# A table of differences on one core: VectorE's subtraction against two products of TensorE into one sum

## What is computed

```python
for t in range(S):
    m_new = np.maximum(f_gate[:, :, t] + m, i_gate[:, :, t])
    f_stab = np.exp(f_gate[:, :, t] + m - m_new)
    i_stab = np.exp(i_gate[:, :, t] - m_new)
    C = f_stab[..., None, None] * C + i_stab[..., None, None] * np.einsum('bhd,bhe->bhde', vt, kt)
    n = f_stab[..., None] * n + i_stab[..., None] * kt
    h_tilde = np.einsum('bhde,bhe->bhd', C, qt)
    denom = np.maximum(np.abs(np.einsum('bhd,bhd->bh', n, qt)[:, :, None]), 1.0)
    y[:, :, t] = o * h_tilde / denom            # o: sigmoid of o_gate
# then, on 1536 tokens of 320 values:
x = rms_norm(y) ; x = (silu(x @ w_gate) * (x @ w_val)) @ w_out      # 320 -> 1536 -> 320
x = leaky_relu(x @ w_in) @ w_out                                    # 320 -> 2048 -> 320
```

## Time and profile before

| | us |
|---|---|
| median of 3 executions | 440.17 (439.88 to 440.44) |
| the profiled execution | 440.19 |
| its span on the core | 438.5 |
| TensorE busy | 429.8 (98%) |
| VectorE busy | 226.3 (52%) |
| ScalarE busy | 193.3 (44%) |
| GpSimd busy | 91.0 (21%) |

### The profile page before, as it was taken

How to read it: one execution, slowest core, us unless ns; L and a number is a source line. 1 busy time by engine, 2 the same in 40 slices (tenths; PEclk the granted TensorE clock), 3 DMA queues, 4 the chain that set the end, 5 groups by cost and what they waited for, 6 DMA issues and landing times.

```text
span 438.5 us, 8229 instructions
## 1 busy us (share of the span) xinstructions
PE 429.8 (98%) x3237; PEld 377.7 (86%) x3237; DVE 226.3 (52%) x439; ACT 193.3 (44%) x428; POOL 91.0 (21%) x97
## 2 busy tenths in 40 slices
PE   7999999999999999999999999999999999999997
PEld 5889999999788888878888888989999999999996
DVE  8856656775466555456433335353333333533534
ACT  4867753665262535235333226553343343333332
POOL 1798852212111111002333004430000000000000
PEclk9999999999999999999999999999999999999999
DMA  7887623431202410001222102300000000100101
GB/s 213 279 294 257 215 86 124 126 121 51 78 27 98 131 47 0 1 1 33 66 67 66 34 1 67 100 0 1 0 1 0 1 1 1 44 17 0 61 0 60
DMA packets 10692, 30.42 MB, mean 69 GB/s; under 512 B 1296, under 2 KB 3264, under 8 KB 10656
## 3 DMA queue, kind: packets, MB, share of 16 engines
q1 hardware_dynamic: 10656, 29.92, 21.4%
HBM read 27.90 MB, written 2.01 MB: 68 GB/s over the span
## 4 chain that ended last, share of the span: by engine, by line
PE 82%; issue 6%; POOL 4%; DMA 4%; DVE 3%; ACT 1%; SPq 0%; POOLq 0%; DVEq 0%
PE gate_ps L1166 22%; PE value_ps L1166 22%; PE out_ps L1243 9%; PE out_ps L1205 9%; PE turn_ps L1243 6%; PE out_ps L1209 3%; PE c_ps L1243 3%; PE turn_ps L1131 3%; POOL w_sb L483 2%; DMA raw<-in_w 2%; PE turn_ps L1092 1%; DMA att_sb<-in_tok 1%; PE turn_ps L1109 1%; PE c_ps L1121 1%; DMA y_acc<-in_first_gates 1%
## 5 line engine op out<-in xcount | busy, mean ns | idle before, releaser
L1166 PE MATMUL value_ps<-x_hi,w_sb 128*128 128x512 f32 (+1 forms) x280 | 68.6, 367 | 0.5 <-DVE h_lo L929 0.5
L1166 PE MATMUL gate_ps<-x_hi,w_sb 128*128 128x512 f32 (+1 forms) x280 | 68.8, 368 | 0.2
L1166 PEld LDWEIGHTS gate_ps<-x_hi,w_sb 128*128 128x128 f32 x280 | 47.4, 191 | 8.2 <-DVE x_odd L895 1.1
L1166 PEld LDWEIGHTS value_ps<-x_hi,w_sb 128*128 128x128 f32 x280 | 47.7, 191 | 7.4 <-DVE h_lo L929 0.7
L908 DVE SCALAR_TENSOR_TENSOR act_buf<-act_buf,gate_ps 128x512 f32<-128x512 f32 (+1 forms) x46 | 26.2, 569 | 48.1 <-ACT act_buf L619 47.9
L934 DVE TENSOR_TENSOR h_lo<-hid,h_hi 128x512 fp32r<-128x512 f32 x48 | 33.2, 692 | 33.7 <-ACT h_hi L638 33.7
L633 ACT ACTIVATE h_hi<-value_ps 128x512 fp32r<-128x512 f32 (+1 forms) x46 | 23.0, 500 | 58.4 <-DVE value_ps L915 58.2
L1205 PE MATMUL out_ps<-h_hi,w_sb 128*128 128x512 f32 (+1 forms) x184 | 48.2, 348 | 0.0
L638 ACT ACTIVATE h_hi<-hid 128x512 fp32r<-128x512 f32 x48 | 30.3, 632 | 37.6 <-DVE hid L922 36.5
L619 ACT ACTIVATE act_buf<-gate_ps 128x512 f32<-128x512 f32 (+1 forms) x46 | 23.1, 501 | 49.3 <-PE gate_ps L1166 49.1
L1243 PE MATMUL out_ps<-w_sb,h_hi 128*128 128x320 f32 x192 | 43.0, 309 | 0.2 <-DVE h_lo L934 0.2
(11 more groups left out here) (148 smaller groups left out, 797.5 us busy)
## 6 DMA issues: line engine op xcount, KB each, us to landing
raw<-in_w SPq DMA_DIRECT2D x12, 544.0 KB, 4.6
att_sb<-in_tok SPq DMA_DIRECT2D x12, 484.0 KB, 4.8
raw<-in_w SPq DMA_DIRECT2D x16, 352.0 KB, 3.0
expo<-decay_scratch SPq DMA_DIRECT2D x10, 512.0 KB, 5.3
att_sb<-in_qk SPq DMA_DIRECT2D x24, 160.0 KB
out_y<-y_acc SPq DMA_DIRECT2D x12, 160.0 KB, 1.9
consts_sb<-in_consts SPq DMA_DIRECT2D x1, 129.5 KB, 2.7
y_acc<-in_first_gates SPq DMA_DIRECT2D x1, 112.0 KB, 2.6
```

Of the source, the lines that this page charges most:

```text
L1166: last = nc.tensor.matmul(ps[:, 0:n], lhs, rhs, start=(j == 0), stop=(j == len(xs) - 1))
```

## The change

It makes a matrix `minus_unit`, the 16x16 unit matrix times -1, on ScalarE. Line 968 goes. On TensorE `difference` takes the place of the second `table`: for each of the five blocks a product with the unit matrix starts a sum and a product of `stab` with `minus_unit` ends it, so the difference is made while the blocks are turned. The wait for `a_done` 4 goes, and one for `minus_set` comes. Block 2 of the weights is loaded before the decays are written out, and `hi_weights(2)` stands before `square(0)`.

```diff
+            minus_unit = sb(first, "minus_unit", [P, NG])
...
@@ SP
             load_raw(1, W1RAW, w1[1, :, :])
+            load_raw(2, W1RAW, w1[2, :, :])
             sp.wait_ge(a_done, 3)
             sp.dma_start(sums[:, 1:, :], by_time[:, 1:, :]).then_inc(scratch_out, 16)
-            load_raw(2, W1RAW, w1[2, :, :])
             sp.wait_ge(scratch_out, 16)
             load_decays(2)
@@ ACT
+            act.wait_ge(consts_in, 16)
+            nc.scalar.activation(minus_unit[0:NG, :], ident_sb[0:NG, 0:NG], ACT.Copy, scale=-1.0).then_inc(minus_set, 1)
             act.wait_ge(tab_ps, 1)
...
             hi_weights(1)
+            hi_weights(2)
             square(0)
-            hi_weights(2)
             square(1)
@@ DVE
-            nc.vector.tensor_tensor(ig[0:NG, rest], ig[0:NG, rest], m, ALU.subtract).then_inc(a_done, 1)
@@ PE
+            def difference(ps, a, b, t0, t1):
+                pe.wait_ge(minus_set, 1)
+                for t in range(t0, t1):
+                    cols = ps[:, (t - t0) * NG:(t - t0 + 1) * NG]
+                    tok = slice(t * P, (t + 1) * P)
+                    nc.tensor.matmul(cols, a[0:NG, tok], ident_sb[0:NG, 0:NG], start=True, stop=False)
+                    last = nc.tensor.matmul(cols, b[0:NG, tok], minus_unit[0:NG, :], start=False, stop=True)
+                last.then_inc(tab_ps, 1)
...
             table(later_a_ps, acum, 1, SEQ_TILES)
-            pe.wait_ge(a_done, 4)
-            table(later_c_ps, ig, 1, SEQ_TILES)
+            difference(later_c_ps, ig, stab, 1, SEQ_TILES)
             update_state(0)
```

More of the change, by code:

```diff
@@ L143, in build @@
             unseen = sb(first, "unseen", [P, P], BF16)
-            used = 4 * (2 * ATT + EXPO * H * P + 2 * H * DV + 6 * DM + 16 + 2 * H + 2 * PAIRS * DV + 3 * TILES * H
+            minus_unit = sb(first, "minus_unit", [P, NG])
+            used = 4 * (2 * ATT + EXPO * H * P + 2 * H * DV + 6 * DM + 16 + NG + 2 * H + 2 * PAIRS * DV + 3 * TILES * H
                         + TILES * PAIRS + 3 * H + 8) + 4 * P
@@ L227, in build @@
         masks_set = sem("masks_set")
+        minus_set = sem("minus_set")
         rows_set = sem("rows_set")
```

## The result

In the comparison, 22 executions of each kernel on the same chips, the kernel before took 440.34 us (median; 439.69 to 440.88) and the changed one **441.59 us** (440.21 to 444.33). The ratio is 1.0042, with a 95% interval of 1.0028 to 1.0056: slower, by 1.25 us, near the 1.4 us forecast. It is a near hit by luck, for a wrong reason, and the 22 times already say so: none lies between 441.89 and 443.42. They fall apart by their mean granted clock. For the kernel before, the clocks on record are those of the 116 executions that were measured beside the experiments; its 22 executions above have none.

A forecast was written before the change was run, and what follows sets the result against it. It took the prologue before `gate(0)` as bound by TensorE and the VectorE/ScalarE path almost together, with a gapless TensorE run behind. Products +1.76 less 0.23 and 0.13 idle gave +1.4; 440.19 + 1.4 = 441.6 us, range 440.1 to 442.4.

The forecast's parts named there:

- Products for transposes: TensorE's second table: five transposes go, ten products (20 records at 0.117 us) come, +1.76 us.
- rival C: The new products are dear: near +4.0 us on TensorE, less 0.36 idle, giving 443.8 us; chance 0.03.
- What is covered: TensorE before `turn(1)`: idle 0.23 us and about 0.13 of turns' waits absorb part of 1.76, leaving +1.4 us.
- rival A: The clock rises sooner relative to `gate(0)`, giving back some or all of the loss (440.9; 439.5 at best); chance 0.19.
- The clock: TensorE's rise from 1.2 to 2.4 GHz, 3.4 us after `gate(0)` starts, shifts along with it and costs nothing.
- Line 968 and the load: Dropping VectorE's subtraction: nothing, at most 0.35 us gained; block 2's load ahead of the decays: nothing.
- Transfers: Decays written near 16.2 us, tile 2's rows landing near 19.7, masked at 20.90: cover 1.2 us, cost nothing.
- The rounding of block 2: On ScalarE ahead of `square(0)`: `normalise(0)` slips 0.1 us at most, covered by 1.4 us; costs 0.1 without cover.
- Rival D: Later tile 2 rows or later blocks reach ScalarE late and hold `h_hi`: up to 1 us more, 442.6; chance 0.06.

The follow-up runs named there:

- the products alone: The changed kernel with block 2's load and rounding back in their old places: 440.81 us, ratio 1.0033.
- filler: The changed kernel with four wide bf16 products, later overwritten, added in TensorE's idle stretches before the table: 443.57 us, ratio 1.0068.

## Why the prediction came out right, and where it was wrong

**Products for transposes: the mis-sized term.** I chose 0.117 us a record "since weight width and moving width both match", from a row of transposes. Measured are 0.213 at 1.2 GHz and 0.112 at 2.4, against 0.117 and 0.06 for a transpose: about 1.8 times at either level. What such a product costs was in a row that I had, line 1092 at 0.23, and I set it aside because it moves 128 columns where these move 16. That width did not matter. A still nearer row stands in the profile of before, a float32 product with a weight of 16x128, at 1.2 GHz:

```profile
6.19 0.42 PE L1074 MATMUL c_ps<-y_acc,consts_sb 16*128 16x128 f32 x1
...
6.83 0.42 PE L1074 MATMUL c_ps<-y_acc,consts_sb 16*128 16x128 f32 x1
```

Three steps of one record lie between them: (6.83 - 6.19) / 3 = 0.213 us, the new records' price. To be a float32 product is not enough: `update_state`'s records are float32 products as well and need 0.049, with weights of 40 columns in place of 128. At 1.2 GHz the term is 20 x 0.213 - 0.59 = +3.7, in place of +1.76. This was rival C, which I gave 0.03 with the words "no row with 16 moving columns is that slow": no row there was a product. Its 443.8 us is what 9 of the 22 executions show (443.88).

The rule that I had set aside fares better. The Trainium skill (FP8 and Floating Point Precision, section TensorE Precision Notes) counts four passes for true FP32. I worked out an estimate of 4.68 us for the ten products from it and set it aside, since a product leaves two records. They took 20 x 0.213 = 4.26 us at 1.2 GHz. So the trace shows two records and not four, but comes near the estimate's total.

**What is covered: right up to `gate(0)`.** The 0.36 us of idle time gave back about what I had put down: 3.3 us worked out, 3.4 measured at `turn(1)` and at `gate(0)` with the products alone. "In the run every wait is relative to TensorE, so nothing is given back" was wrong. In that profile `gate(0)` is 23.90 - 20.54 = 3.4 us late, `gate(5)` 42.87 - 39.97 = 2.9, and so is the end (441.4 - 438.5). The rise did not shift along with `gate(0)`, as I had assumed. It comes at about 25.1, in the two records of 24.92 that take 0.49 us, 1.2 us behind `gate(0)`; in the kernel before it came 3.4 us behind. That is rival A's mechanism, worth 0.5 us here. Only from there on is the run rigid: from `gate(5)` to the end it is 398.5 us in the profile before (438.5 - 39.97) and 398.6 in that after (439.0 - 40.42).

**The clock: the step that failed.** "The small products from 11.93 to 17.45 did not raise it" held for the one execution that I read. In 63 of 116 executions of the kernel before the mean clock says that it rose early. So an early rise was no novelty of the change, as rival A had it, but the more frequent case of both kernels. With it the products cost 20 x 0.112 = 2.24, where five transposes took 0.3: +1.9 on TensorE. The idle 0.85 and 0.23 us of TensorE take up more than half of it. In the profile with the load alone moved, `gate(0)` starts at 20.37 and `gate(4)` at 35.32; in the changed kernel's at 20.79 and 35.93. The loss is 0.4 us at the start of the run and 0.6 by its fifth block, and the medians of the groups differ by 0.8.

**The median, then,** is that of 13 executions with an early rise, which lose some 0.8, and 9 which lose 3.6; the 1.4 in between is the cost in neither group. With other shares the median would have been another: the products alone, with 8 to 4, have theirs at 440.81, outside the forecast's own 441.1 to 442.2. That 441.6 was met is luck. Whether the change itself shifts the shares is open: 13 of 22 and 63 of 116 do not differ.

**Line 968 and the load: nothing, right**, by the runs without the subtraction and with the load alone. `minus_unit` has no run of its own.

**Transfers: right.** The decays are issued at 10.16 and written 5.6 us later, at 15.8 (forecast 16.2); their rows for tile 2, issued at 15.74, land 3.7 us later at 19.4 (forecast 19.7), and GpSimd masks them at 20.85, as before.

**The rounding of block 2: right in the changed kernel, too small on its own.** The block is rounded from 15.54, `square(1)` starts at 17.10 (17.16 before) and `normalise(0)` slips by 0.14 us, where I wrote "0.1 at most". The products cover it. "With the cover gone it would cost the 0.1" was wrong: without the products `turn(0)` waits 0.33 us with the load moved too, and 0.65 with the rounding alone, where the block is only rounded from 15.93.

**Rival D, transfers**, is partly real, but as far as the runs tell it is not the change's. The changed kernel's profile has a block that ScalarE waits 2.85 us for:

```profile
35.33 1.11 ACT L616 ACTIVATE w_sb<-raw 128x1088 fp32r<-128x1088 f32 x1 [2.85 <-DMA raw<-in_w]
```

From `gate(4)` to `gate(5)` it takes 40.42 - 35.93 = 4.49 us, and 39.38 - 35.32 = 4.06 with the load alone moved: 0.4 us of this profile's 1.1 us of longer span (439.0 against 437.9) comes there. Both profiles of the kernel before have a wait at the same place (2.34 and 2.14 us), and 4.06 us from `gate(4)` to `gate(5)`. So a wait of 2.3 us costs nothing there, and one of 2.85 costs 0.4. That looks like scatter; that the change has no part in it is argued, from the load alone costing nothing, and not shown.

**Open:** what decides, in an execution, whether the clock rises early. The filler was one try at it and failed. Open too is what makes the fall behind it 6.8 us long in some and 3.4 in others. Those are the slow ones: both executions of the kernel before above 442 us, and the one of each of the kernels with only the load and only the rounding moved, have a mean clock of 0.992.

## What to carry to other kernels

Price a new float32 product by the row of a float32 product with as wide a weight, at the same clock level, and not by a transpose with the same tile shapes. Here it made no difference whether 16 or 128 columns moved. Where the only such row looks too dear, ask which property of it really differs. Before you take a clock's history from a profile, look at the executions' times and mean clocks: one profile shows one history, and a median may stand between two groups of executions in neither of which it is the cost. A product can be the same work as a transpose and a subtraction, but if its engine is the one that sets the end, moving work there from a half-idle one needs a price before anything else.

## What the runs showed of the hardware

- A float32 product's record with a weight of 16x128 and 16 moving columns is 0.213 us from the next at 1.2 GHz and 0.112 at 2.4; a product leaves two of them. With 128 moving columns it is 0.213 at 1.2 GHz as well (line 1074). A transpose of the same block is one record of 0.117 and 0.06.
- The clock can rise, fall and rise again within ten microseconds: 2.4 GHz from 15.8 to 19.2 us, 1.2 to 22.6, then 2.4. By the mean clock the kernel before rises early in 63 of 116 executions, with 0.991 to 0.992 in 15 of these; in the two profiles at 0.992 the fall is longer (6.8 us without the subtraction). In the changed kernel's profile the clock rose behind 3.6 us of gapless products of 41 columns and five transposes, and fell behind a stretch in which TensorE was busy without a gap (3.40 of 3.40 us).
- The record of the granted clock reads 1.00 before its first event. In the stretch from 12 to 15.8 us it did so while the work ran at 1.2 GHz; only the durations of equal forms show the level there.
- Four more wide bf16 products ahead of that work did not make the rise surer (3 of 6 executions, against 13 of 22).
